# Rounding and lower part of g made in the step of their own product, ahead of the couples' work

## What is computed

```python
X = np.fft.rfft(x, axis=1)                      # x: 4 x 3008 x 256
Yr = Xr @ w_r - Xi @ w_i + b_r
Yi = Xr @ w_i + Xi @ w_r + b_i
Yr, Yi = soft_shrink(Yr, 0.01), soft_shrink(Yi, 0.01)
y = np.fft.irfft(Yr + 1j * Yi, n=3008, axis=1)
h = y.reshape(12032, 256) @ w_in                # 256 x 2048
g = np.maximum(h, 0) + alpha * np.minimum(h, 0)
out = g @ w_out                                 # 2048 x 256
```

## Time and profile before

| | |
|---|---|
| median of 3 runs | 1435.1 us (1433.63 to 1435.76) |
| the profiled execution, its own time | 1435.66 us |
| its span, first to last instruction | 1433.7 us, 21627 instructions |
| PE busy | 96% of the span |
| PE weight loads | 1158.0 us, 81% |
| DVE busy | 1000.2 us, 70% |
| ACT busy | 771.9 us, 54% |
| POOL busy | 294.3 us, 21% |
| DMA | 106.83 MB, mean 75 GB/s |
| granted TensorE clock, mean | 0.991 of full |

### The profile page before, as it was taken

The page is one execution under the profiler, slowest core; times in us unless marked ns, Lnnn a source line. Parts: engine busy times, 40 slices in busy tenths (PEclk is TensorE's granted clock), DMA queues, the critical chain, the costliest instruction groups (busy, mean ns, idle before and its releaser), DMA issues. The chain is left out here.

```text
span 1433.7 us, 21627 instructions
## 1 busy us (share of the span) xinstructions
PE 1375.3 (96%) x6890; PEld 1158.0 (81%) x6890; DVE 1000.2 (70%) x1887; ACT 771.9 (54%) x1708; POOL 294.3 (21%) x354
## 2 busy tenths in 40 slices
PE   6999999998999999999999999999999999999997
PEld 3987788887888888887888888888788888888886
DVE  5775777887866657877876666777786666566654
ACT  3775555655644545555654455565564544444433
POOL 1433432222201422212210242122220100001000
PEclk9998999999999999999999999999999999999999
DMA  7754432221211542313212243232220211012101
GB/s 223 196 150 135 147 88 68 73 75 55 74 43 32 145 119 58 77 53 88 64 37 56 57 133 85 59 82 70 59 67 26 48 37 37 23 37 48 26 16 15
DMA packets 175856, 106.83 MB, mean 75 GB/s; under 512 B 113224, under 2 KB 151416, under 8 KB 175744
## 3 DMA queue, kind: packets, MB, share of 16 engines
q1 hardware_dynamic: 170938, 100.92, 26.3%
q10 hardware_dynamic: 4806, 4.54, 1.0%
HBM read 67.87 MB, written 37.49 MB: 73 GB/s over the span
## 5 line engine op out<-in xcount | busy, mean ns | idle before, releaser
L1038 DVE SCALAR_TENSOR_TENSOR g_raw<-negpart,keep,h_ps 128x502 f32<-128x502 f32 (+1 forms) x384 | 282.4, 735 | 301.1 <-ACT negpart L810 294.4
L810 ACT ACTIVATE negpart<-h_ps 128x502 f32<-128x502 f32 (+1 forms) x384 | 225.7, 588 | 405.8 <-PE h_ps L475 405.2
L475 PE MATMUL out_ps<-g_hi,wout_hi 128*128 128x502 f32 (+1 forms) x768 | 307.9, 401 | 30.3 <-DVE g_lo L937 28.7
L475 PE MATMUL h_ps<-y_hi,win_hi 128*128 128x502 f32 (+1 forms) x768 | 304.5, 397 | 1.6 <-DVE y_lo L1027 1.3
L475 PE MATMUL h_ps<-y_lo,win_hi 128*128 128x502 f32 (+1 forms) x768 | 300.8, 392 | 0.0
L475 PE MATMUL out_ps<-g_hi,wout_lo 128*128 128x502 f32 (+1 forms) x768 | 300.3, 391 | 0.0
L475 PE MATMUL h_ps<-y_hi,win_lo 128*128 128x502 f32 (+1 forms) x768 | 299.8, 390 | 0.0
L475 PE MATMUL out_ps<-g_lo,wout_hi 128*128 128x502 f32 (+1 forms) x768 | 299.6, 390 | 0.0
L937 DVE TENSOR_TENSOR g_lo<-g_raw,g_hi 128x502 fp32r<-128x502 f32 (+1 forms) x384 | 267.1, 696 | 0.1
L819 ACT ACTIVATE g_hi<-g_raw 128x502 fp32r<-128x502 f32 (+1 forms) x384 | 236.5, 616 | 2.7 <-DVE g_raw L1038 2.5
L475 PEld LDWEIGHTS out_ps<-g_hi,wout_hi 128*128 128x128 f32 x768 | 144.6, 188 | 73.1 <-DVE g_lo L937 40.4
(11 more groups left out here) (126 smaller groups left out, 1990.9 us busy)
## 6 DMA issues: line engine op xcount, KB each, us to landing
pair_raw<-fwd_scratch SPq DMA_DIRECT2D x96, 128.0 KB, 2.2
back_raw<-inv_scratch SPq DMA_DIRECT2D x61, 192.0 KB, 2.4
table<-in_twiddles_dram SPq DMA_DIRECT2D x28, 384.0 KB, 3.5
x_raw<-in_x_dram SPq DMA_DIRECT2D x64, 160.0 KB
inv_scratch<-inv_sb SPq DMA_DIRECT2D x36, 256.0 KB, 2.2
fwd_scratch<-staging SPq DMA_DIRECT2D x44, 192.0 KB, 2.1
inv_sb<-inv_scratch SPq DMA_DIRECT2D x122, 64.0 KB, 2.4
out_dram<-turned SPq DMA_DIRECT2D x124, 40.0 KB, 1.8
```

The source lines that it names most:

```text
L475: mm = pe.matmul(ps, lhs, rhs, start=(first and n == 0), stop=(last and n == len(terms) - 1), **kw)
L810: act.activation(negpart[:, q % 2, 0:size], h_ps[:, q % 2, 0:size], ACT.Relu, scale=-1.0).then_inc(negpart_done, 1)
L1038: dve.scalar_tensor_tensor(g_raw[:, q % 2, 0:size], negpart[:, q % 2, 0:size], keep[:, m:m + 1], h_ps[:, q % 2, 0:size], ALU.mult, ALU.add ...
```

## The change

In the loop of ACT, `split_bent` is called for the step's own product (q) instead of the last one (q-1), and stands behind copy_fwd, split_mixw, split_pair, split_back and split_tw, ahead of above_couple. In the loop of DVE, `rest_bent` is called for q instead of q-1, and stands behind turn, split_x, rest_pair and rest_first, ahead of shrink_couple. The two calls behind the loops, for the last step, go. No other order, no buffer and no wait inside a function is changed; PE, POOL and SP have the same programs.

```diff
--- before.py
+++ after.py
@@ -885,9 +885,6 @@
             for f in range(TILES):
                 for m in range(STEPS):
                     bend(f, m)
-                    q = f * STEPS + m
-                    if q >= 1:
-                        split_bent(*divmod(q - 1, STEPS))
                     s = s_unit(f, m)
                     if s is not None:
                         copy_fwd(s)
@@ -902,6 +899,7 @@
                     p = p_unit(f, m, -3)
                     if p is not None and p % 3 == 0:
                         split_tw(p // 3)
+                    split_bent(f, m)
                     p = p_couple(f, m, 3)
                     if p is not None:
                         above_couple(p)
@@ -927,7 +925,6 @@
                     p = p_couple(f, m, 5)
                     if p is not None:
                         copy_couple(p)
-            split_bent(TILES - 1, STEPS - 1)
             for n in range(1, 12, 2):
                 store_out(act, TILES - 1, n)
 
@@ -1139,9 +1136,6 @@
             for f in range(TILES):
                 for m in range(STEPS):
                     bend(f, m)
-                    q = f * STEPS + m
-                    if q >= 1:
-                        rest_bent(*divmod(q - 1, STEPS))
                     if f >= 1 and m == LAG - 1:
                         turn(f - 1, 0)
                         turn(f - 1, 1)
@@ -1153,6 +1147,7 @@
                     v = i_bpair(f, m - 2)
                     if v is not None:
                         rest_first(v)
+                    rest_bent(f, m)
                     p = p_couple(f, m, 3)
                     if p is not None:
                         shrink_couple(p)
@@ -1173,7 +1168,6 @@
                     u = i_unit(f, m)
                     if u is not None:
                         rest_y(u)
-            rest_bent(TILES - 1, STEPS - 1)
             turn(TILES - 1, 0)
             turn(TILES - 1, 1)
```

## The result

The changed kernel takes 1482.9 us (median of 4, 1482.64 to 1485.07) against 1435.2 of the kernel before in the same comparison: ratio 1.0337, interval 1.0320 to 1.0355, so 48 us slower. The forecast was 1455 with a range up to 1475: the direction came as forecast, and the chain of ACT and DVE as the new bound too; the size did not. The profiled execution has a span of 1483.0 us, 49.3 over the one before.

What follows compares the result with a forecast made beforehand. Prediction: PE bounds the kernel before; the ACT-DVE chain would bound the three stretches after. Stretches +22.9, first tile -2.3, tail -0.6: in all +20 on 1435.7, about 1455 us; own range 1440 to 1470, full range up to 1475.

Steps and rivals of the forecast that it cites:

- What bounds it: Stretches (54 steps with units, one per period): PE's wait for g_lo, up to 28.7 us, goes; DVE becomes the bound.
- Rival A: PE stays the bound in the stretches and the 28.7 us of waits for g_lo go: 1407 us, chance 0.10.
- The hole: On DVE between g_raw and g_lo: g_lo starts 0.77 us later every step, adding 24.4 us per stretch after deductions.
- What DVE has to spare: DVE's idle ahead of g_raw, 21.8 us a stretch: 13.3 absorbs the hole, plus 2.0 of overlap; chain 221.2 us.
- The "full" steps: 12 steps of a stretch, 9 with rest_first and 3 with turn, fill DVE's hole: cost 0.
- The credit at a stretch's end: PE takes over with 2.7 us of lateness forgiven instead of 0.65: -2.0 us per stretch.
- Light steps and period starts: Steps without units are covered by PE, and copy_fwd and x_hi fill the hole in period starts: cost nothing.
- The tail: At the end, output(382) no longer waits for g_lo(382), and the last output waits as now: -0.6 us.
- The point at which nothing would change: Under rival B, each stretch must lose 7.7 of the 24.4 us for no change: a hole of about 0.55 us.
- B: ACT's own lateness, 8.5 us of DVE idle per stretch, is absorbed too: 1430 us, chance 0.17.
- C: PE's granted clock falls in each of 18 groups of nine steps, costing 27 us more: 1482 us, chance 0.08.
- D: The couples' results, such as spec_lo for mix_couple, reach PE late, costing 43 us: 1498 us, chance 0.05.

Runs made afterwards that it cites:

- the variant with earlier units: Changed kernel with every inverse1, split_y and rest_y one step earlier in its tile: 1479.0 us, ratio 1.0327 to the kernel before.
- its second run: The changed kernel run again, unaltered, beside three of its variants: 1482.4 us, ratio 1.0336 to the kernel before.
- The woven kernel: Changed kernel with split_bent moved behind above_couple and copy_more on ACT, rest_bent behind whole_spec on DVE: 1402.5 us, ratio 0.9784 to the kernel before.

## Why the prediction was wrong in size, point by point

**What bounds it.** Right. The wait for g_lo went (28.7 to 2.4), and the ACT-DVE chain became the bound of the stretches; outside of them and of the first tile PE stayed it. Rival A, which the rule of the Trainium skill ("Perfetto Trace Analysis", Identifying the Most-Contended Engine) had on its side, fell. LDWEIGHTS busy share is 76% against DVE's 74% in the second stretch after, and neither is what bounds it: occupancy doesn't count waits inside a chain of two engines.

One sign didn't come. PE was to wait for g_raw ahead of hidden, and did so for 0.4 us in the second stretch. What it waits for there is y_lo (6.3 us ahead of hidden, 3.8 ahead of inverse1), inv_sb (4.8) and spec_lo (2.5): the chain's lateness reaches PE through the other products of DVE and ACT, and the tolerance that was worked out for g_raw isn't the one that counts.

**The hole.** Right to 0.01 us: 1.42 from g_raw to g_lo, 0.77 later than before. The count, 26 empty and 16 half-filled, is the 42 waits of the trace. 23.7 us of idle, plus 0.08 that each wait takes from the overlap of two instructions, is 27.1; 26.6 were priced, before the 1.5 taken off. Counted by steps, each without the idle ahead of its next g_raw, the 26 took 17.9 us more and the 16 took 7.1, together 25.0; 25.1 were priced.

**What DVE has to spare**, the step that failed in the stretches. It said that 13.3 of the 21.8 us of idle ahead of g_raw would be absorbed, with 2.0 more from overlap, and that a full hole costs 0. The chain was to be 221.2 us and was 227.7 to 229.2, on average 7.2 more.
- 12.3 us of idle stayed instead of 8.5, so 9.5 were absorbed and not 13.3. Two of the idles that stayed, 1.58 and 0.92 us, end two steps of the second stretch (3.67 and 5.77 us, where the variant with earlier units has 2.39 and 4.50). There PE can't be ahead of DVE over a tile's edge, because hidden of the next tile needs y_lo of step 14, and with that wait the clock falls to half; without the half clock, 0.22 of the 1.58 would be left. The tolerance of 2.7 us that I had worked out from a light step doesn't hold there. The variant took off 2.1 us a stretch.
- The overlap counted once for the 8 idles that went, 0.6 us, and not 25 times.
- The "full" steps weren't free: with rest_first ahead, g_lo runs beside POOL's back_lo, 1.10 us instead of 0.68 (610.40 for one). g_lo is 1.8 us longer a stretch, back_hi 1.1 and shrunk 0.4 shorter, and the nine steps with rest_first take 1.4 us more in all; the three with turn did cost nothing. That this is contention was tested in the first tile alone; here it is read from the rows.
- 0.7 was taken off for mix_mm; it was 0.4.

Together 3.8 + 1.4 + 1.4 + 0.3 = 6.9 of the 7.2. The credit at a stretch's end was 1.0 a period (57.7 to 56.7), where 2.0 stood, and 0.4 of it is the tile edge's.

**Light steps and period starts**, "cost nothing": right where PE bounds, wrong in the first tile, the second step of the prediction that failed. The sentence that copy_fwd and x_hi fill the hole had DVE's and ACT's work in view and left out what x_hi sets off: x_lo on POOL, just when g_lo runs. -2.3 was forecast, +5.4 came, and moving split_x alone gave 6 us back.

**Not priced**: turn now stands ahead of g_lo on DVE, so output of the new tile's first step waits less for it. This is 0.3 to 0.4 us at each light tile edge (the step from m = 2 took 3.06 us and takes 2.75), and most of the 3.2 us gained in the last period and the two later period starts.

**The tail**, -0.6: right.

The point at which nothing would change was worked out wrongly too: for a sum of 0, each stretch had to lose 20 / 3 = 6.7 of the 24.4 us, over 42 steps 0.16 each, which is a hole of about 0.61 and not 0.55. No result hangs on it.

In sum, forecast +22.9 - 2.3 - 0.6 = +20. Measured, 50.5 - 3.1 = +47.4 in the stretches with their ends, +5.4 in the first tile, -3.2 at tile edges and -0.6 at the end: +49. Of the 29 that are missing, 24.5 are the stretches' and 7.7 the first tile's, against 3.2 gained.

**The rivals.** B (ACT's lateness is absorbed) fell: 12.3 us of idle stayed. C came true in part: the granted clock is 0.98 to 0.99 in the stretches instead of 0.99 to 1.00, with six falls to half in them instead of two, each at a wait of 3.1 to 3.2 us, so in lumps. At the first of the two tile edges of a stretch this lies on the path, for 1.4 us in one step of the second stretch and perhaps as much in the next; at the other edge the two steps (4.21 and 3.83 us) are as long as in the variant with earlier units (4.22 and 3.83), which has no fall there. As an estimate from these steps, C is worth 0.6 to 2.5 of the 16.8 us that a stretch lost, where it had priced 9. D: PE did wait for spec_lo, 7.5 us in all, longest 0.7; the terms above leave no room for its price.

**The range**, up to 1475, took the holes as the only thing unsure. The bounds should have come from the terms set at nothing: the full steps, the first tile, the edge of a tile.

## What to carry to other kernels

When two engines hand work to and fro, an operation whose operand is fresh costs the wait that it makes on its own engine and the delay of what the other engine needs next; the second can be the larger (moved alone, ACT's half, which leaves DVE no hole, cost 38 us, and the whole change 48). Don't only ask whether it may stand earlier, but which existing wait of its engine it can fill: here the same two calls, a few lines further down, turned 3.3% slower into 2.2% faster. And for each instruction that is moved, look at what it sets off on a third engine, and what then runs beside it.

## What the runs showed of the hardware that was not expected

A DVE subtraction of 128x502 with both operands in SBUF takes 0.68 us alone, 1.10 beside one POOL instruction of back_lo, 1.55 beside one of x_lo (1.29 us on POOL), and 3.59 beside several in a row. Both long ones end 0.54 us after an instruction of POOL does (142.87 + 1.55 against 142.59 + 1.29, and 146.15 + 3.59 against 147.93 + 1.27), and so do all 85 of the 384 g_lo that take over 1.0 us in the changed kernel, within 0.01 us: as if DVE got hardly anything through until POOL was done. Each of the 85 starts while POOL runs; which reads or writes of POOL hold it up was not tested. Whose instruction bears this is a matter of the order alone: before the change, rest_first (1.77 us at 141.50) and rest_win (2.36 at 143.30) bore it in the first tile, in a step of 6.54 us; in the changed kernel g_lo with its 3.59 bears it, in a step of 6.56, and it is the step behind it that differs (2.89 us instead of 1.57).

All six waits of PE of over 3 us in the stretches of the changed kernel came with a fall of the granted clock to half, within the wait or up to 1.0 us behind it. So did the six of its second run and the six of the variant with split_x behind rest_bent, there up to 1.2 us behind. The woven kernel, where no wait of PE in the stretches is over 0.8 us, has none.
